# A routing count and its threshold moved half a block later in TensorE's order

## Chip, cores and metric

The kernel runs on 1 core of one Trainium2 chip. The metric is the device time in microseconds of one execution, the median over several. Engines: TensorE (PE, with PEld for its weight loads), VectorE (DVE), ScalarE (ACT), GpSimd (POOL) and SyncE (SP).

## Reference

Three stages. The first is a gated recurrence over 768 steps for 4 x 8 heads of width 40. It gives x of 3072 tokens x 320. The second routes and computes experts, the third is a two-layer network with ELU:

```python
logits = x @ w_gate                      # 3072 x 8
order = np.argsort(-logits.flatten())    # greedy, cap = 384 tokens per expert
for idx in order:
    tok, e = int(idx) // E, int(idx) % E
    if assigned[tok] >= 0 or counts[e] >= cap: continue
    assigned[tok] = e; counts[e] += 1
...
out[mask] = np.maximum(x[mask] @ w1[e], 0.0) @ w2[e]      # 320 -> 1024 -> 320
...
h = x @ w_in                                              # 320 -> 2048
g = np.where(h > 0.0, h, np.exp(np.minimum(h, 0.0)) - 1.0)
return (g @ w_out).astype(np.float32)                     # 2048 -> 320
```

## The kernel before

The recurrence (first 183 us or so of the execution) is untouched by the change. After it, the experts are filled one after another: each turn k of 0 to 7 finds the expert that is full next, computes its 384 tokens through both networks, and meanwhile does the routing for the turns behind it. "First expert" is turn 0, "steady" turns are the others. `after` is min(7 - k, 2), so that `after == 2` holds for k = 0 to 5.

A turn has two halves. In the first, TensorE does `up` and `down` for 8 blocks of 128 hidden features (W1, W2). In the second it runs over f = 0 to 18. Block f does `up2(k, f)` for f below 16 (eight products of 384 columns with the two parts of w_in, into a bank of PSUM) and, three blocks behind, `down2(k, f - 3)` (nine products of 320 columns with the two parts of w_out, from `gl_hi` and `gl_lo`). In between, `up2`'s output passes ScalarE (`elu_tanh` and `elu_exp`: relu L1681, tanh L1684, exponential L1693), VectorE (`elu`: L1503, L1506), ScalarE again (`elu_hi`: L1700, gl_hi) and GpSimd (`elu_lo`: L1243, gl_lo). `up2(k, f)` waits for `elu(k, f - 2)`, `down2(k, f - 3)` for `gl_lo` of its own block.

The routing for turn c + 1 = k + 2 is a search for a threshold, in six rounds, which runs inside these blocks:

- a comparison on VectorE (`cmp`): for the first round in six slices (`compare_first`, L849), laid behind `elu` of f = 0 to 4; for later rounds `round_compare` (L1326).
- a count on TensorE: `count_takers` (L1768), 24 products of 8 columns into bank 7.
- a test on VectorE (`round_test`: L1339, L1341), which gives `feas`.
- the spreading of the threshold on TensorE: `count_thresholds` (L1788), one product.
- the move of the threshold on VectorE (`round_move`, L1348, writes `base`), and then the next round's comparison.

Rounds 2 to 5 use `count_parts` (L1774) and `fold_parts` (L1782) instead of one count. Each engine executes its instructions in the order in which its function writes them out by hand, and waits on semaphores where data come from another engine. A wait holds everything behind it on that engine. `count_beside(k)` is the block at which the first round's count and spreading stand: 7 for the first expert, 5 for steady ones.

Of the kernel before, what the change touches and what calls it, by code (L numbers as in the profile page):

```python
# [956 lines left out]
def experts(nc, ctx, sem, bank, t, pieces, tables, E, G, CAP, DM, FF, FF2, XK):  # L957
# [155 lines left out]
    def first_expert(k):  # L1113
        return isinstance(k, int) and k == 0
# [58 lines left out]
    def count_beside(k):  # L1173
        return 7 if first_expert(k) else 5
# [97 lines left out]
    def _(dve):  # L1272
# [17 lines left out]
        def keys_at(k):  # L1290
            return (B - 1 + k) * KEY_STEPS
# [14 lines left out]
        def compare_first(k, part):  # L1306
            n = G // SLICES
            ins = tables.first_compare(dve, tables.ramp1_p, slice(part * n, part * n + n), n, keys_at(k))
            if part == SLICES - 1:
                ins.then_inc(cmp_ok, 1)  # L1310
# [24 lines left out]
        def round_test(k, q):  # L1335

            n = STEPS[q - 1][1]
            dve.wait_ge(count_pe, k * ROUNDS + q)
            nc.vector.tensor_tensor(over[0:n, :], pR[0:n, 0:E], rem[0:n, :], ALU.is_ge).then_inc(r_step, 1)  # L1339
            dve.wait_ge(r_step, did(k))  # L1340
            nc.vector.tensor_reduce(feas[0:n, :], over[0:n, :], AX.X, ALU.max).then_inc(feas_ok, 1)  # L1341
# [198 lines left out]
        def body(k, s, n, after):  # L1540

            c = k + 1
            for u in range(2, NF):
                if first_expert(k):
                    if u == 2:
                        finish_round(1, 1)
                        round_compare(1, 2)
                        round_parts(1, 2)
                        hidden(0, 2)
                        round_test(1, 2)  # L1550
                        round_move(1, 2)
                        round_compare(1, 3)
                    elif u == 3:
                        round_parts(1, 3)
                        hidden(0, 3)
                        round_test(1, 3)
                        round_move(1, 3)
                        round_compare(1, 4)
                        finish_round(1, 4)
                        round_compare(1, 5)  # L1560
                    elif u == 4:
                        round_parts(1, 5)
                        hidden(0, 4)
                        round_test(1, 5)
                        round_move(1, 5)
                        round_compare(1, 6)
                        finish_round(1, 6)
                        choose_counts(1)
                    elif u == 5:
                        choose_expert(1)  # L1570
                        hidden(0, 5)
                    elif u == 6:
                        choose_ties(1)
                        hidden(0, 6)
                    else:
                        hidden(0, 7)
                        choose_leave(1)
                        choose_close(1)
                    continue
                if after:  # L1580
                    if u == 2:
                        choose_counts(c)
                    elif u == 3:
                        choose_expert(c)
                    elif u == 4:
                        choose_ties(c)
                    elif u == 5:
                        choose_leave(c)
                        choose_close(c)
                    elif u - 6 in range(2):  # L1590
                        choose_spots(c, 2 * (u - 6))
                        choose_spots(c, 2 * (u - 6) + 1)
                hidden(k, u)
            if after == 2 and not first_expert(k):
                choose_start(c + 1)
            between_layers(k)
            for f in range(NF2):
                q, odd = (f - rounds_behind(k)) // 2 - 1, f % 2
                if after == 2:
                    if f == 0:  # L1600
                        if first_expert(k):
                            choose_start(c + 1)
                        choose_keys(c + 1)
                    if f == count_beside(k):
                        round_test(c + 1, 1)
                    elif f == count_beside(k) + 1:
                        round_move(c + 1, 1)
                        round_compare(c + 1, 2)
                    if q >= 2 and odd:
                        if q in FOLDED:  # L1610
                            round_parts(c + 1, q)
                        else:
                            round_test(c + 1, q)
                    elif q > 2:
                        round_move(c + 1, q - 1)
                        round_compare(c + 1, q)
                elu(k, f)
                if after == 2 and odd and q in FOLDED:
                    round_test(c + 1, q)
                if after and not first_expert(k) and f == list_beside(k):  # L1620
                    choose_tokens(c, 1 - s, n + s)
                if after == 2:
                    for part in (SLICES_BESIDE_SPOTS if first_expert(k) else SLICES_BESIDE).get(f, ()):
                        compare_first(c + 1, part)
                if first_expert(k) and 1 <= f <= SPOTS:
                    choose_spots(c, f - 1)
                if first_expert(k) and f == list_beside(k):
                    choose_tokens(c, 1 - s, n + s)
                if TURN <= f < TURN + NJ and after:
                    columns(c, f - TURN)  # L1630
            if first_expert(k):
                round_move(c + 1, ROUNDS - 1)
                round_compare(c + 1, ROUNDS)
                hidden(c, 0)
                round_test(c + 1, ROUNDS)
                hidden(c, 1)
            elif after:
                hidden(c, 0)
                hidden(c, 1)
            if after == 2:  # L1640
                round_move(c + 1, ROUNDS)
# [116 lines left out]
    def _(pe):  # L1758
# [197 lines left out]
        def body(k, s, n, after):  # L1956
            c = k + 1
            for u in range(2, NF):
                up(k, u)
                later = 2 if first_expert(k) else 0  # L1960
                if later and u == 2:
                    count_thresholds(1, 1)
                elif later and u < 5:
                    one_round(1, 2 * u - 3)
                if after:
                    if u == 3 + later:
                        totals(c)
                    elif u == 4 + later:
                        prefix(c, 1, eqs)
                down(k, u - 2)  # L1970
                if later and u < 5:
                    one_round(1, 2 * u - 2)
                if u == 5 + later and after:
                    prefix(c, 2, mem)
            down(k, NF - 2)
            down(k, NF - 1)
            for f in range(NF2 + LAG):
                if f == 0:
                    up2_first_two(k)
                elif 1 < f < NF2:  # L1980
                    if f == LAG and after and not first_expert(k):
                        list_tokens(c)
                    up2(k, f)
                q = (f - rounds_behind(k)) // 2 - 1
                routing = after == 2 and f < NF2 + rounds_behind(k) and q >= 2
                if after == 2 and f == count_beside(k):
                    count_takers(c + 1, 1)
                    if first_expert(k):
                        list_tokens(c)
                elif routing and f % 2:  # L1990
                    (count_parts if q in FOLDED else count_takers)(c + 1, q)
                elif routing and q - 1 in FOLDED:
                    count_thresholds(c + 1, q - 1)
                if f >= LAG:
                    down2(k, f - LAG)
                if after == 2 and f == count_beside(k):
                    count_thresholds(c + 1, 1)
                elif routing and f % 2:
                    (fold_parts if q in FOLDED else count_thresholds)(c + 1, q)
                if TURN <= f < TURN + NJ and after:  # L2000
                    columns(c, f - TURN)
                if NF2 <= f < NF2 + 2 and after:
                    up(c, f - NF2)
        experts_in_turn(pe, body)


# [22 lines left out]
```

## Time and profile before

| | |
|---|---|
| median of 3 runs | 837.94 us (837.02 to 840.19) |
| the profiled execution, its own time | 841.97 us |
| its span, first to last instruction | 840.3 us |
| mean granted TensorE clock | 0.987 |
| busy: TensorE, VectorE, ScalarE, GpSimd | 794.3, 524.4, 466.6, 392.7 us |

Busy time is the time in which an engine has an instruction in execution. Matmuls overlap each other, so the distance from the start of one to the start of the next, not its duration, is what a stream of them costs. An idle time in brackets behind a row is that of the engine just before the instruction, with what ended it.

### The profile page before, as it was taken

The page shows a single profiled execution, that of the slowest core. Times are in us where ns is not written, and L with a number is a line of the kernel's source. Part 1 is how long each engine was busy: PE and PEld are TensorE (multiplying, and loading weights), DVE is VectorE, ACT ScalarE, POOL GpSimd, SP SyncE. Part 2 cuts the span into 40 slices and gives each one's busy share as a digit, 9 for nine tenths or more (in the row PEclk, how much of TensorE's full clock was granted, in tenths as well). Part 3 has the DMA queues.
Part 4 walks back from the last instruction along what each step waited for, and adds up shares of the span by engine and source line. Part 5 has one row for each costly group of instructions (what it writes and reads, how often), then busy time and mean ns, then how long its engine had stood idle before and what let it go on. Part 6 is the DMA issues. An engine that isn't in the chain of part 4 may idle for free.

```text
span 840.3 us, 17700 instructions
## 1 busy us (share of the span) xinstructions
PE 794.3 (95%) x6029; PEld 741.3 (88%) x6029; DVE 524.4 (62%) x1438; ACT 466.6 (56%) x990; POOL 392.7 (47%) x466
## 2 busy tenths in 40 slices
PE   5999999989979999999999999999999999999994
PEld 5899999987768889899989989998999899999894
DVE  5566776766768567665866585576658656542441
ACT  5445545422417663785478276728835772893672
POOL 3535454454623652465076345516552662664133
PEclk9999999999999999999999999999999999999998
DMA  4999999413410212111122201121211212121000
GB/s 78 142 154 178 151 169 171 100 57 112 124 53 26 84 48 68 46 55 55 44 69 62 69 26 60 48 68 47 71 55 45 69 48 68 47 70 39 2 1 23
DMA packets 137987, 60.96 MB, mean 73 GB/s; under 512 B 104696, under 2 KB 136184, under 8 KB 137912
## 3 DMA queue, kind: packets, MB, share of 16 engines
q1 hardware_dynamic: 135608, 52.13, 28.7%
q0 software_dynamic: 2304, 7.87, 2.9%
q8 instruction: 42, 0.69, 0.3%
q14 instruction: 33, 0.27, 0.1%
HBM read 51.67 MB, written 8.26 MB: 71 GB/s over the span
## 4 chain that ended last, share of the span: by engine, by line
PE 63%; DVE 9%; ACT 3%; issue 1%; POOL 1%; DMA 0%; ACTq 0%; POOLq 0%
PE bank L1825 7%; PE bank L1910 7%; PE bank L1826 6%; PE bank L1828 6%; PE bank L1912 6%; PE bank L1911 6%; PE bank L1830 3%; PE bank L1829 3%; PE bank L1868 3%; PE bank L1866 3%; PE bank L1867 3%; PE bank L1762 2%; DVE cmp L849 2%; DVE unit L1506 2%; DVE unit L1503 2%
## 5 line engine op out<-in xcount | busy, mean ns | idle before, releaser
L1243 POOL TENSOR_TENSOR gl_lo<-unit,gl_hi 128x384 fp32r<-128x384 f32 x128 | 130.3, 1018 | 274.3 <-ACT gl_hi L1700 274.2
L1910 PE MATMUL bank<-Wo_hi,gl_hi 128*128 128x320 f32 x384 | 125.6, 327 | 0.5 <-POOL gl_lo L1243 0.5
L1912 PE MATMUL bank<-Wo_hi,gl_lo 128*128 128x320 f32 x384 | 119.3, 311 | 0.0
L1911 PE MATMUL bank<-Wo_lo,gl_hi 128*128 128x320 f32 x384 | 119.2, 310 | 0.0
L1503 DVE SCALAR_TENSOR_TENSOR unit<-bank,unit 128x384 f32<-128x384 f32 x104 | 57.8, 555 | 84.2 <-ACT bank L1693 79.3
L1664 ACT ACTIVATE hid_hi<-bank 128x384 fp32r<-128x384 f32 x64 | 31.4, 491 | 127.5 <-PE bank L1830 127.5
L1681 ACT ACTIVATE unit<-bank 128x384 f32<-128x384 f32 x128 | 62.2, 486 | 62.8 <-PE bank L1830 53.5
L1825 PE MATMUL bank<-x_hi,Wi_hi 128*128 128x384 f32 x224 | 81.3, 363 | 2.4 <-DVE unit L1506 1.6
L1826 PE MATMUL bank<-x_hi,Wi_lo 128*128 128x384 f32 x224 | 76.6, 342 | 0.0
L1910 PEld LDWEIGHTS bank<-Wo_hi,gl_hi 128*128 128x128 f32 x384 | 73.2, 191 | 3.1 <-POOL gl_lo L1243 3.1
L1506 DVE TENSOR_TENSOR unit<-unit,bank 128x384 f32<-128x384 f32 x128 | 70.9, 554 | 4.4
L1911 PEld LDWEIGHTS bank<-Wo_lo,gl_hi 128*128 128x128 f32 x384 | 72.9, 190 | 0.0
L1912 PEld LDWEIGHTS bank<-Wo_hi,gl_lo 128*128 128x128 f32 x384 | 72.8, 190 | 0.0
L1486 DVE SCALAR_TENSOR_TENSOR hid_lo<-bank,hid_hi 128x384 fp32r<-128x384 f32 x64 | 35.4, 554 | 55.3 <-ACT hid_hi L1664 55.1
L1684 ACT ACTIVATE unit<-unit 128x384 f32<-128x384 f32 x128 | 67.3, 525 | 4.0
L1700 ACT CAST gl_hi<-unit 128x384 fp32r<-128x384 f32 x128 | 63.9, 499 | 3.9 <-DVE unit L1506 3.5
L366 POOL TENSOR_SCALAR_AFFINE_SELECT W<-W 128x512 f32<-128x512 f32 x48 | 33.3, 716 | 66.7 <-ACT W L579 66.7
L1828 PE MATMUL bank<-x_lo,Wi_hi 128*128 128x384 f32 x224 | 58.0, 340 | 0.0
L1693 ACT ACTIVATE bank<-unit 128x384 f32<-128x384 f32 x104 | 51.5, 495 | 3.0
L501 DVE TENSOR_TENSOR PW<-bank,W 128x512 f32<-128x512 f32 x48 | 30.9, 686 | 25.8 <-PE bank L649 21.1
L695 PE MATMUL bank<-v_in,PW 128*128 128x96 f32 x384 | 46.8, 275 | 0.0
L1825 PEld LDWEIGHTS bank<-x_hi,Wi_hi 128*128 128x128 f32 x224 | 42.9, 192 | 3.6 <-DVE unit L1506 3.6
(289 smaller groups left out, 2125.6 us busy)
## 6 DMA issues: line engine op xcount, KB each, us to landing
stage<-in_moe_w_dram SPq DMA_DIRECT2D x32, 320.0 KB, 2.9
stage<-in_moe_w_dram SPq DMA_DIRECT2D x32, 256.0 KB, 2.6
stage<-in_moe_w_dram SPq DMA_DIRECT2D x96, 64.0 KB, 2.4
k_in<-in_k_dram SPq DMA_DIRECT2D x24, 160.0 KB, 3.6
q_in<-in_q_dram SPq DMA_DIRECT2D x24, 160.0 KB, 4.2
o_in<-in_o_gate_dram SPq DMA_DIRECT2D x24, 160.0 KB, 4.1
v_in<-in_v_dram SPq DMA_DIRECT2D x24, 160.0 KB, 3.6
x_rows<-xt SPq DMA_DIRECT2D x24, 160.0 KB, 3.3
```

What stands on the lines that cost most here:

```text
L1243: nc.gpsimd.tensor_tensor(gl_lo[:, b, :], ex[:, b, :], gl_hi[:, b, :].bitcast(F32), ALU.subtract).then_inc(gl_ok, 1)
L1503: nc.vector.scalar_tensor_tensor(out=ex[:, b, :], in0=exp_at(f), scalar=1.0, in1=th[:, f % 2, :], op0=ALU.add, op1=ALU.mult).then_inc(em_o ...
L1506: nc.vector.tensor_tensor(ex[:, b, :], ex[:, b, :], ring[(NF + f) % 3][:, 0:CAP], ALU.max).then_inc(g_ok, 1)
L1681: nc.scalar.activation(ex[:, b, :], ring[(NF + f) % 3][:, 0:CAP], ACT.Relu, scale=-1.0).then_inc(neg_ok, 1)
L1684: nc.scalar.activation(th[:, f % 2, :], ex[:, b, :], ACT.Tanh, scale=-0.5).then_inc(th_ok, 1)
L1700: nc.scalar.copy(gl_hi[:, b, :], ex[:, b, :]).then_inc(gl_hi_ok, 1)
L1825: nc.tensor.matmul(to, w_hi[:, c, cols], x_hi[m][:, c, :], start=(c == 0), stop=False)
L1826: nc.tensor.matmul(to, w_lo[:, c, cols], x_hi[m][:, c, :], start=False, stop=False)
L1828: nc.tensor.matmul(to, w_hi[:, c, cols], x_lo[m][:, c, :], start=False, stop=False)
L1910: nc.tensor.matmul(acc[j][:, 0:DM], gl_hi[:, f % RG, t_], Wo_hi[:, f, :], start=(f == 0), stop=False)
L1911: nc.tensor.matmul(acc[j][:, 0:DM], gl_hi[:, f % RG, t_], Wo_lo[:, f, :], start=False, stop=False)
L1912: ins = nc.tensor.matmul(acc[j][:, 0:DM], gl_lo[:, f % RG, t_], Wo_hi[:, f, :], start=False, stop=(f == NF2 - 1))
```

## The change

In steady turns with `after == 2` (k = 1 to 5), the first count stands behind `down2(k, 2)` instead of ahead of it, in block f = 5, and the spreading stands in block f = 6, behind `up2(k, 6)` and ahead of `down2(k, 3)`, instead of at the end of block 5. On VectorE the test moves from ahead of `elu(k, 5)` to behind it. The move of the threshold and the comparison of round 2 keep their place, ahead of `elu(k, 6)`. The first expert keeps its order.

```diff
@@ VectorE
                     if f == count_beside(k):
-                        round_test(c + 1, 1)
+                        if first_expert(k):
+                            round_test(c + 1, 1)
                     elif f == count_beside(k) + 1:
                         round_move(c + 1, 1)
                         round_compare(c + 1, 2)
...
                     for part in (SLICES_BESIDE_SPOTS if first_expert(k) else SLICES_BESIDE).get(f, ()):
                         compare_first(c + 1, part)
+                    if f == count_beside(k) and not first_expert(k):
+                        round_test(c + 1, 1)
@@ TensorE
-                if after == 2 and f == count_beside(k):
+                if after == 2 and first_expert(k) and f == count_beside(k):
                     count_takers(c + 1, 1)
-                    if first_expert(k):
-                        list_tokens(c)
+                    list_tokens(c)
+                elif after == 2 and not first_expert(k) and f == count_beside(k) + 1:
+                    count_thresholds(c + 1, 1)
                 elif routing and f % 2:
...
                 if f >= LAG:
                     down2(k, f - LAG)
                 if after == 2 and f == count_beside(k):
-                    count_thresholds(c + 1, 1)
+                    (count_thresholds if first_expert(k) else count_takers)(c + 1, 1)
```

## Rows read from the trace of the kernel before

**Rows 1.** The page, part 1: busy us, share of span, instructions.

```profile
PE 794.3 (95%) x6029; PEld 741.3 (88%) x6029; DVE 524.4 (62%) x1438; ACT 466.6 (56%) x990; POOL 392.7 (47%) x466
```

**Rows 2.** Waits of TensorE, 330 to 700 us: total us, times, longest.

```profile
PE bank L1768 <- DVE cmp L849: 8.0, 5, 1.6
```

**Rows 3.** Chain of waits at expert 2: start us, us, what.

```profile
425.63 0.60 DVE cmp L849
...
426.28 0.76 PE bank L1768 x24
```

**Rows 4.** Timeline of expert 2, 422 to 435 us: start us, us, engine, line.

```profile
422.41 1.02 POOL L1243 TENSOR_TENSOR gl_lo<-unit,gl_hi 128x384 fp32r<-128x384 f32 x1
...
424.37 0.34 PE L1830 MATMUL bank<-x_lo,Wi_hi 128*128 128x384 f32 x1
...
425.55 0.67 DVE L849 SCALAR_TENSOR_TENSOR cmp<-hi,bank 128x508 bf16<-128x508 f32 x1
425.86 0.49 ACT L1693 ACTIVATE bank<-unit 128x384 f32<-128x384 f32 x1
...
426.28 0.76 PE L1768 MATMUL bank<-pick,cmp 128*128 128x8 bf16 x24 [1.57 <-DVE cmp L849]
...
426.90 0.39 PE L1910 MATMUL bank<-Wo_hi,gl_hi 128*128 128x320 f32 x1
...
427.27 0.16 DVE L1341 TENSOR_REDUCE feas<-over 127x1 bf16<-127x8 f32 x1
427.35 0.55 DVE L1503 SCALAR_TENSOR_TENSOR unit<-bank,unit 128x384 f32<-128x384 f32 x1
...
428.31 0.18 PE L1788 MATMUL bank<-feas,first 128*128 128x1 bf16 x1
428.34 0.42 PE L1825 MATMUL bank<-x_hi,Wi_hi 128*128 128x384 f32 x1
428.53 0.16 DVE L1348 TENSOR_SCALAR base<-bank 128x1 f32<-128x1 f32 x1
...
428.73 0.99 DVE L1326 SCALAR_TENSOR_TENSOR cmp<-hi,base,bank 128x744 bf16<-128x744 f32 x1
...
429.66 0.34 PE L1830 MATMUL bank<-x_lo,Wi_hi 128*128 128x384 f32 x1
429.83 0.31 PE L1910 MATMUL bank<-Wo_hi,gl_hi 128*128 128x320 f32 x1
...
431.11 0.49 ACT L1693 ACTIVATE bank<-unit 128x384 f32<-128x384 f32 x1
431.16 0.34 PE L1825 MATMUL bank<-x_hi,Wi_hi 128*128 128x384 f32 x1
...
434.26 0.42 PE L1825 MATMUL bank<-x_hi,Wi_hi 128*128 128x384 f32 x1
```

**Rows 5.** Timeline of TensorE: count and later up2, experts 1 and 3.

```profile
349.53 0.78 PE L1768 MATMUL bank<-pick,cmp 128*128 128x8 bf16 x24 [1.59 <-DVE cmp L849]
...
355.88 0.34 PE L1825 MATMUL bank<-x_hi,Wi_hi 128*128 128x384 f32 x1
...
501.55 0.76 PE L1768 MATMUL bank<-pick,cmp 128*128 128x8 bf16 x24 [1.59 <-DVE cmp L849]
...
507.96 0.34 PE L1825 MATMUL bank<-x_hi,Wi_hi 128*128 128x384 f32 x1
```

**Rows 6.** Windows behind the five counts: length, busy per engine, granted clock, DMA.

```profile
350.00:353.30 3.30, 3.30 (x24) 3.10 (x21) 1.62 (x6) 0.97 (x3) 2.10 (x3) 0.50 0.22 63
...
426.90:430.20 3.30, 3.30 (x27) 3.20 (x24) 2.50 (x6) 0.99 (x3) 1.97 (x3) 1.00 0.26 81
503.60:506.90 3.30, 3.30 (x13) 3.30 (x13) 1.31 (x3) 0.31 (x1) 0.53 (x1) 0.50 0.46 134
578.90:582.20 3.30, 3.30 (x28) 3.20 (x26) 2.50 (x6) 0.98 (x3) 2.00 (x3) 1.00 0.24 81
654.20:657.50 3.30, 3.30 (x29) 3.20 (x26) 2.49 (x6) 0.98 (x3) 2.00 (x3) 1.00 0.24 77
```

## The prediction

> **What bounds the kernel now.** I read the page first: TensorE is busy for 794.3 of 840.3 us [rows 1], so it is nearly always the engine that decides, and a change can win only where TensorE stands still or runs at a lower clock. The list of waits on TensorE over experts 1 to 5 and their neighbourhood (330 to 700 us) then holds a single entry: five waits of the first count (L1768) for the comparison on VectorE (L849), 8.0 us together, 1.6 us the longest [rows 2]. These five are the count that the diff moves, one for each expert from 1 to 5. Nothing else in this half of the kernel makes TensorE wait. The chain of waits agrees: at expert 2 it runs through VectorE's last comparison slice and then into the count [rows 3].
>
> The timeline of expert 2 shows why [rows 4]. The eight products of up2 for f = 5 issue their last at 424.37 us. The count is next in TensorE's order, but it needs the last slice of the comparison, which VectorE can only start at 425.55, behind its ELU work of f = 4, and which takes 0.67 us to 426.22. So the count starts at 426.28, after 1.57 us of idle time. The next item, the nine products of down2 for f = 2, needed only gl_lo of f = 2, which GpSimd had finished at 422.41 + 1.02 = 423.43. It is ready work standing behind a wait.
>
> A second loss sits right behind the wait. At experts 1 and 3 the granted clock is 0.50 (1.2 GHz) for some 3.3 us after it, and at experts 2, 4 and 5 it stays at 1.00 (2.4 GHz) in the same place [rows 6]. From the start of the count to the start of up2 for f = 7 are 431.16 - 426.28 = 4.88 us at expert 2, but 355.88 - 349.53 = 6.35 at expert 1 and 507.96 - 501.55 = 6.41 at expert 3 [rows 4, 5]. A fall thus costs 1.5 us.
>
> **The count, moved behind down2.** No instruction is added or removed. There are 24 count products, one spreading product, the nine of down2 and eight of up2 before and after, and no DMA is issued by the moved steps. What changes is the order. down2 for f = 2 would start 0.17 us behind the last product of up2 (the distance from 429.66 to 429.83), at 424.54, and its input has been there for 1.1 us. A down2 takes 431.16 - 429.83 = 1.33 us from its first start to that of the next stage [rows 4]. So TensorE is through with it at 425.87, its last product drains to about 426.0, and the count still starts at 426.28: VectorE's slice is not touched by the move. About 0.26 us of the 1.57 us wait remain, and up2 for f = 6 follows at 426.90, where down2 started before. The move is worth 1.33 us per expert: the whole down2, since it lies inside the wait.
>
> **The spreading, moved behind up2 of f = 6.** It now waits for the test on VectorE, and the test is moved behind ELU of f = 5. Before, VectorE stood idle in front of the test, and ELU of f = 5 (whose exponential was ready at 425.86 + 0.49 = 426.35) began only at 427.35. Now ELU starts at about 426.4 and takes at most the 1.18 us between 427.35 and 428.53, to 427.6. The count is done at 427.04 and waits for no one. Test and reduction take what they take now, 427.27 + 0.16 - 427.04 = 0.39 us, so the flag is there at 427.96. up2 for f = 6 runs 429.83 - 428.34 = 1.49 us from 426.90 to 428.39. The spreading is then 0.43 us behind its flag and waits for nothing. Its own cost, 0.03 us on TensorE (428.31 to 428.34), is unchanged [rows 4].
>
> **What the moved spreading makes late.** On VectorE the move of the threshold (L1348) and the second comparison (L1326) stand ahead of ELU of f = 6, and are queued behind a result that now comes later relative to up2. Threshold: 428.39 + 0.22 (428.31 to 428.53 now) = 428.61. The comparison starts 0.20 later and takes 0.99: done at 429.80. Everything on ScalarE for f = 6 follows up2's end, now 428.34 - 426.90 = 1.44 us sooner, so its exponential ends at 431.60 - 1.44 = 430.16. The comparison is out of the way 0.36 us before ELU could begin. If it were not, ELU ending at 430.16 + 1.18 = 431.34 would still be early for its reader, up2 for f = 8, at 434.26 - 1.33 = 432.93: another 1.59 us of cover. The second count, behind up2 of f = 7 (at about 431.2), finds its comparison done for 1.4 us. So this half of the edit costs nothing, with that cover. Bounds: nothing below, and above it the 1.33 us it could at most give back per expert before it does harm [rows 4].
>
> **Sum.** 5 x 1.33 = 6.65 us. up2 for f = 7 then starts at 426.28 + 0.62 + 1.49 + 0.03 + 1.41 = 429.83 instead of 431.16 (0.62 from the count's to the next start, 1.41 for a down2 behind small products, 426.90 to 428.31): the same 1.33, by another way.
>
> **The clock.** Both falls follow the longest quiet stretch of TensorE in the block: 1.59 us idle, then 24 products of 8 columns [rows 5, 6]. Behind the change only about 0.26 us of idle time stands ahead of the count, so I expect these falls to go: 2 x 1.5 = 3.0 us in the profiled execution, 0 if they stay. For that execution, 841.97 us (its span of 840.3 and 1.67 around it), the sum is 6.65 + 3.0 = 9.65, giving 832.3. The timed median is 837.94, 4.0 lower, and its three runs spread over 3.17 us, about two falls. So a timed run has probably fewer falls than the profiled one. I take one, between the bounds of none and two: 837.94 - 6.65 - 1.5 = 829.8. With none to save it is 831.3, with two 828.3.
>
> The Trainium skill, "TensorE: Matmul & The Clock Gate", What's actually happening, calls the throttled clock the default that activity releases, and the two levels in the rows are its two. But its section "Why this matters for your kernels" warns only of idle gaps longer than any of these five. Read so, the falls were not due to these waits and would stay: 831.3, the first rival.
>
> **Rivals.** (1) The falls stay or were not in the timed runs: 837.94 - 6.65 = 831.3. For it: three of the five waits had no fall. Against: both falls came right behind this wait. (2) The saved time is given back at the next wait, because ELU and gl_lo cannot follow a TensorE that is never idle. Then the wait moves to up2 or down2 of f = 7 or 8, and the result is 837.94, or 836.4 with one fall less. For it: the exponential of f = 6 ends at 431.60 and ELU 1.18 later, 3.1 us behind the last product of its up2 (429.66), more than the 1.49 + 1.33 = 2.8 us of one block on TensorE. Against: its reader comes two blocks later, VectorE stands idle from 429.72 to 431.6, and the covers worked out above are 0.4 to 1.6 us [rows 4]. (3) Slower: VectorE, in order, stands at the threshold's move in front of ELU of f = 6, and up2 for f = 8 starves. The result would have to reach VectorE 0.36 + 1.59 + 1.33 = 3.28 us later than I reckon to eat the gain, and 0.84 us more in each of the five experts to be 0.5% slower: 842.1. It takes 0.22 us now, so little speaks for it. (4) The change does nothing, as down2 would wait for gl_lo of f = 2 as long as the count does for its comparison. It decides from 1.1 us of lateness; 837.9, and counted with (2).
>
> **How the numbers follow.** Forecast 0.72; rival 1: 0.18; rivals 2 and 4: 0.07; rival 3: 0.03. The forecast and rival 1 together span 828.3 to 831.3 by the number of falls; with the spread of a median of such runs, some 1 us below and 1.7 us above for a part given back, the range is 827.3 to 833.0. Half a per cent is 4.2 us, about what the measurement can tell from no change, so faster means below 833.7. The forecast and rival 1 are faster: 0.90; rivals 2 and 4 within: 0.07; rival 3 slower: 0.03.
>
> **What would show it.** Right: five waits of L1768 for L849 of about 0.25 us, 1.3 us in all instead of 8.0; down2 of f = 2 starting 0.17 us behind up2; no wait at L1788; no wait of up2 or down2 for f = 7 and 8; ELU of f = 5 about 0.95 us sooner after its comparison slice; the granted clock at 1.00 throughout experts 1 to 5. Wrong: down2 of f = 2 waiting for gl_lo, VectorE reaching ELU of f = 6 later than its exponential, the first count later than 0.06 us behind the comparison, or a fall of the clock still behind the count.

## The result, and the profile after

| | before | after |
|---|---|---|
| median | 837.61 us (837.02 to 840.19, 4 runs) | 830.02 us (828.95 to 830.4, 4 runs) |
| profiled execution, its own time | 841.97 us | 828.95 us |
| its span | 840.3 us | 827.2 us |
| mean granted TensorE clock in it | 0.987 | 0.996 |

The ratio after to before is 0.9901, with a 95% interval of 0.9879 to 0.9924: 7.6 us faster. The forecast started from 837.94 (three runs) and took 8.15 us off. With the fourth run the median before is 837.61, and 7.59 us came off.

The line numbers of VectorE and GpSimd named here stay, TensorE's and ScalarE's are three higher after the change: the count is L1771 (was L1768), the spreading L1791 (was L1788), up2 L1828 to L1833, down2 L1913 to L1915.

The waits of TensorE in the kernel after, 330 to 690 us (total us, times, longest), which answer to [rows 2]:

```profile
PE bank L1771 <- DVE cmp L849: 1.4, 5, 0.3
```

Still one entry, still five times, but 1.4 us in all where it was 8.0. Its first place, expert 1, in the timeline of the kernel after (start us, us, engine, line), which answers to [rows 4]:

```profile
342.10 1.02 POOL L1243 TENSOR_TENSOR gl_lo<-unit,gl_hi 128x384 fp32r<-128x384 f32 x1
...
344.04 0.34 PE L1833 MATMUL bank<-x_lo,Wi_hi 128*128 128x384 f32 x1
...
344.21 0.31 PE L1913 MATMUL bank<-Wo_hi,gl_hi 128*128 128x320 f32 x1
...
345.23 0.68 DVE L849 SCALAR_TENSOR_TENSOR cmp<-hi,bank 128x508 bf16<-128x508 f32 x1
345.38 0.31 PE L1915 MATMUL bank<-Wo_hi,gl_lo 128*128 128x320 f32 x1
...
345.97 0.76 PE L1771 MATMUL bank<-pick,cmp 128*128 128x8 bf16 x24 [0.28 <-DVE cmp L849]
...
346.08 0.56 DVE L1503 SCALAR_TENSOR_TENSOR unit<-bank,unit 128x384 f32<-128x384 f32 x1 [0.17 <-ACT bank L1696]
...
346.58 0.42 PE L1828 MATMUL bank<-x_hi,Wi_hi 128*128 128x384 f32 x1
...
347.33 0.17 DVE L1341 TENSOR_REDUCE feas<-over 127x1 bf16<-127x8 f32 x1
...
348.08 0.18 PE L1791 MATMUL bank<-feas,first 128*128 128x1 bf16 x1
348.12 0.39 PE L1913 MATMUL bank<-Wo_hi,gl_hi 128*128 128x320 f32 x1
...
348.31 0.16 DVE L1348 TENSOR_SCALAR base<-bank 128x1 f32<-128x1 f32 x1 [0.81 <-PE bank L1791]
...
348.51 0.99 DVE L1326 SCALAR_TENSOR_TENSOR cmp<-hi,base,bank 128x744 bf16<-128x744 f32 x1
...
349.52 0.34 PE L1828 MATMUL bank<-x_hi,Wi_hi 128*128 128x384 f32 x1
...
349.89 0.56 DVE L1503 SCALAR_TENSOR_TENSOR unit<-bank,unit 128x384 f32<-128x384 f32 x1 [0.39 <-ACT bank L1696]
```

down2 of f = 2 starts 0.17 us behind the last product of up2 (344.04 to 344.21) and fills the hole. Its gl_lo had been there since 342.10 + 1.02 = 343.12. The count still starts 0.06 us behind the end of the slice (345.23 + 0.68 = 345.91). The idle time ahead of it is 0.28 us. The spreading waits for nothing: its flag is there at 347.50, it starts at 348.08. From the count to up2 of f = 7 it is 349.52 - 345.97 = 3.55 us.

How much each expert gained is read best from one count to the next. Two rows of the kernel after, experts 1 and 3, on TensorE's timeline:

```profile
345.97 0.76 PE L1771 MATMUL bank<-pick,cmp 128*128 128x8 bf16 x24 [0.28 <-DVE cmp L849]
...
493.90 0.76 PE L1771 MATMUL bank<-pick,cmp 128*128 128x8 bf16 x24 [0.27 <-DVE cmp L849]
```

That is (493.90 - 345.97) / 2 = 73.97 us per expert. Before, where the clock stayed up, it is 501.55 - 426.28 = 75.27 us [rows 4, 5]. The move took 1.30 us out of each expert, 6.5 us out of five.

The two profiled spans differ by 13.1 us, much more than the medians. Most of the rest goes with the clock. Before, the fall at experts 1 and 3 cost 1.5 us each [rows 4, 5, 6], and three more falls stood in parts that the change leaves alone. Windows of the kernel before (the number behind the engines is the granted clock):

```profile
22.40:25.60 3.20, 3.20 (x16) 2.85 (x17) 0.16 (x1) 2.22 (x5) 0.69 (x2) 0.50 0.41 49
278.40:281.70 3.30, 3.30 (x12) 3.10 (x12) 2.38 (x7) 0.07 (x1) 0.04 (x1) 0.50 0.44 139
182.80:186.10 3.30, 3.30 (x12) 3.30 (x12) 2.20 (x11) 0.72 (x1) 0.52 (x2) 0.50 0.64 199
```

and the same stretches in the kernel after, with the clock up in all three:

```profile
22.40:25.60 3.20, 2.35 (x21) 2.14 (x22) 0.54 (x2) 2.42 (x5) 0.99 (x2) 1.00 0.40 44
183.00:186.30 3.30, 3.30 (x23) 3.14 (x23) 2.23 (x12) 0.47 (x1) 0.58 (x2) 1.00 0.62 197
276.00:279.30 3.30, 3.29 (x22) 3.03 (x21) 2.59 (x7) 1.19 (x3) 0.26 (x1) 1.00 0.51 139
```

The first moved count comes 349.53 - 345.97 = 3.56 us earlier than before, all of it won ahead of the first instruction that the change moves. The fall at 22.4 us has no share in it: behind the recurrence the products with `Wi_hi` (L1762, after the change L1765) start at 182.56 before and at 182.82 after. The first count behind them comes at 187.52 and 186.19, so the fall at 182.8 cost 0.26 + 1.33 = 1.6 us. By the first expert's count the lead is 276.03 - 273.81 = 2.22 us, which is 0.9 more, and whose cause was not followed. The last 1.34 us come in the stretch with the fall at 278.4. So 13.1 = 3.56 (ahead of the change) + 6.5 (the move) + 3.0 (the falls at experts 1 and 3). How much of a timed run's gain is falls is a question of its own, which the experiments take up.

### The profile page after: what moved, and what is told of

Same layout as the page of the kernel before. It is cut to its first block, busy times and chain, and to the rows that moved or that the text cites. A ratio compares the mean times of both kernels' runs of the same rounds, so it can differ in the third digit from the quotient of the medians.

```text
span 827.2 us, 17700 instructions
## 1 busy us (share of the span) xinstructions
PE 787.0 (95%) x6029; PEld 733.8 (89%) x6029; DVE 524.2 (63%) x1438; ACT 467.4 (56%) x990; POOL 393.4 (48%) x466
## 4 chain that ended last, share of the span: by engine, by line
PE 63%; DVE 6%; ACT 5%; issue 2%; POOL 1%; DMA 0%; ACTq 0%; POOLq 0%
PE bank L1828 7%; PE bank L1913 7%; PE bank L1829 6%; PE bank L1831 6%; PE bank L1915 6%; PE bank L1914 6%; PE bank L1833 3%; PE bank L1832 3%; PE bank L1869 3%; PE bank L1871 3%; PE bank L1870 3%; PE bank L1765 2%; PE bank L1857 1%; DVE unit L1506 1%; PE bank L1854 1%
## 5 line engine op out<-in xcount | busy, mean ns | idle before, releaser
L1913 PE MATMUL bank<-Wo_hi,gl_hi 128*128 128x320 f32 x384 | 124.8, 325 | 0.6 <-POOL gl_lo L1243 0.6
L1915 PE MATMUL bank<-Wo_hi,gl_lo 128*128 128x320 f32 x384 | 118.6, 309 | 0.0
L1828 PE MATMUL bank<-x_hi,Wi_hi 128*128 128x384 f32 x224 | 80.2, 358 | 2.4 <-DVE unit L1506 1.6
L1913 PEld LDWEIGHTS bank<-Wo_hi,gl_hi 128*128 128x128 f32 x384 | 72.5, 189 | 3.1 <-POOL gl_lo L1243 3.1
L1915 PEld LDWEIGHTS bank<-Wo_hi,gl_lo 128*128 128x128 f32 x384 | 72.1, 188 | 0.0
L945 POOL TENSOR_TENSOR W_lo<-stage,W_hi 128x512 fp32r<-128x512 f32 x32 | 41.4, 1293 | 9.4 <-ACT W_hi L936 9.3
```

Of the source, the lines that this page charges most:

```text
L1828: nc.tensor.matmul(to, w_hi[:, c, cols], x_hi[m][:, c, :], start=(c == 0), stop=False)
L1913: nc.tensor.matmul(acc[j][:, 0:DM], gl_hi[:, f % RG, t_], Wo_hi[:, f, :], start=(f == 0), stop=False)
L1915: ins = nc.tensor.matmul(acc[j][:, 0:DM], gl_lo[:, f % RG, t_], Wo_hi[:, f, :], start=False, stop=(f == NF2 - 1))
```

## Experiments

The kernels below ran in sets of four, each set on a chip of its own, beside the kernel before. A median alone tells little here: in the second set one unchanged kernel spread from 836.72 to 845.31 us. Most of that goes with the mean granted clock of the run. Over the 157 runs whose clock is on record (all but the four of the kernel before in the first table), a straight line with one slope and an offset for each kernel gives 6.3 us more for a mean clock lower by 0.01, and leaves 0.9 us of scatter. The table gives the median, the mean over runs of the granted clock, the time that this line gives at a mean clock of 0.990, and from the trace the distance from one expert to the next at full clock (between the moves of the first round's threshold, L1348). The 75.29 us of the kernel before are from its first trace; the values of hole_longer have falls in them.

| kernel | runs | median us | ratio to before, 95% | clock | us at 0.990 | us per expert |
|---|---|---|---|---|---|---|
| before, set 1 | 23 | 840.62 | | 0.990 | 839.8 | 75.29 |
| count_only, set 1 | 12 | 834.61 | 0.9925 (0.9896 to 0.9955) | 0.991 | 835.1 | 74.47 |
| spread_only, set 1 | 12 | 839.97 | 1.0003 (0.9974 to 1.0032) | 0.990 | 840.1 | 75.28 |
| slice_before, set 1 | 6 | 830.33 | 0.9884 (0.9845 to 0.9923) | 0.991 | 831.4 | 73.63 |
| slice_after, set 1 | 6 | 829.31 | 0.9876 (0.9833 to 0.9920) | 0.989 | 829.7 | 73.52 |
| before, set 2 | 23 | 841.07 | | 0.989 | 839.9 | |
| after_again, set 2 | 6 | 832.67 | 0.9918 (0.9890 to 0.9946) | 0.989 | 832.6 | 73.98 |
| fill_before, set 2 | 12 | 840.60 | 1.0009 (0.9986 to 1.0032) | 0.989 | 840.0 | 75.29 |
| delay1, set 2 | 6 | 829.85 | 0.9896 (0.9862 to 0.9930) | 0.992 | 832.5 | 73.98 |
| delay3, set 2 | 12 | 838.04 | 0.9976 (0.9953 to 0.9999) | 0.992 | 840.2 | 75.53 |
| before, set 3 | 11 | 837.13 | | 0.992 | 839.5 | |
| hole_longer, set 3 | 6 | 849.15 | 1.0139 (1.0108 to 1.0170) | 0.983 | 845.5 | 77.2 to 77.7 |
| hole_filled, set 3 | 6 | 844.82 | 1.0080 (1.0051 to 1.0109) | 0.991 | 845.5 | 76.44 |
| test_first, set 3 | 6 | 831.88 | 0.9926 (0.9899 to 0.9954) | 0.989 | 831.5 | 73.97 |
| slice_again, set 3 | 6 | 829.97 | 0.9907 (0.9877 to 0.9936) | 0.990 | 830.6 | 73.51 |

The changed kernel as first measured (830.02, mean clock 0.995) comes out at 833.0 by the same line, after_again at 832.6. Against before, at one clock, that is 7 us, close to the 6.5 of the traces.

**The change in two halves: count_only.**

```diff
 VectorE, against the changed kernel
-                        if first_expert(k):
-                            round_test(c + 1, 1)
+                        round_test(c + 1, 1)
...
-                    if f == count_beside(k) and not first_expert(k):
-                        round_test(c + 1, 1)
 TensorE
-                elif after == 2 and not first_expert(k) and f == count_beside(k) + 1:
-                    count_thresholds(c + 1, 1)
...
-                    (count_thresholds if first_expert(k) else count_takers)(c + 1, 1)
+                    if not first_expert(k):
+                        count_takers(c + 1, 1)
+                    count_thresholds(c + 1, 1)
```

> The count stands behind down2 of f = 2 as in the changed kernel, but the spreading follows it at once, in block 5, and VectorE's test stays ahead of ELU of f = 5. Theory (the gain is the down2 laid into the wait, and the spreading had to go half a block later to keep it): TensorE waits for the test behind the count, about 0.4 us idle and 0.6 us from start to start, so 0.7 of the 1.33 us per expert remain, 3.6 us in all: 834.0 without a change in clock falls, 833 to 834. A wait of L1788 for L1341 of about 0.4 us shows in five places. Rival (the move of the spreading is idle detail): as the changed kernel, 830.0.

Measured: 834.61 us, 74.47 us per expert, so 0.82 of the 1.31 us remain (0.7 was expected). VectorE's test has its old place here too, which test_first below shows to be without effect. TensorE's waits in this kernel, 330 to 720 us:

```profile
PE bank L1788 <- DVE feas L1341: 2.3, 5, 0.5
PE bank L1768 <- DVE cmp L849: 1.4, 5, 0.3
```

The count's wait is as short as in the changed kernel, and a new one of 0.46 us stands five times at the spreading. The second half of the edit is there to keep the first half's gain.

**spread_only.**

```diff
 TensorE, against the changed kernel
-                if after == 2 and first_expert(k) and f == count_beside(k):
+                if after == 2 and f == count_beside(k):
                     count_takers(c + 1, 1)
-                    list_tokens(c)
+                    if first_expert(k):
+                        list_tokens(c)
...
-                if after == 2 and f == count_beside(k):
-                    (count_thresholds if first_expert(k) else count_takers)(c + 1, 1)
+                if after == 2 and first_expert(k) and f == count_beside(k):
+                    count_thresholds(c + 1, 1)
```

> The count keeps its old place ahead of down2 of f = 2; only the spreading goes behind up2 of f = 6 and the test behind ELU of f = 5. Theory: nothing is gained and nothing lost, 837.6 within 1 us, five waits of 1.6 us for the comparison as before. Rival (VectorE's freed order is what pays, since ELU of f = 5 no longer stands behind the test): several us faster. Rival (the late threshold holds up ELU of f = 6): slower by some 1 us per expert.

Measured: ratio 1.0003, 75.28 us per expert where the clock stayed up, and the five waits of before (8.0 us, 5 times). The later spreading and the freed VectorE give nothing by themselves and cost nothing. (The time of 837.6 that was expected is missed by the level of this set, whose kernel before stood at 840.62.)

**test_first**, the changed kernel with VectorE's old place for the test:

```diff
 VectorE, against the changed kernel
-                        if first_expert(k):
-                            round_test(c + 1, 1)
+                        round_test(c + 1, 1)
...
-                    if f == count_beside(k) and not first_expert(k):
-                        round_test(c + 1, 1)
```

> The changed kernel with VectorE's test of the first round back ahead of ELU of f = 5. Theory (that place matters to no one, because ELU of f = 5 has its reader a block later and the flag is wanted only behind up2 of f = 6): VectorE waits for the count 0.7 us again, TensorE does not; period from expert to expert 73.98 us as in the changed kernel. Rival (VectorE's idle time is what the change removed): 1 us per expert slower.

Measured: 73.97 us per expert, as in the changed kernel, and the waits of TensorE are the same 1.4 us in five places. ELU of f = 5 had room; where the test stands on VectorE is free.

**Another cure for the same wait: slice_before and slice_after.** The same line in the kernel before and in the changed one:

```diff
-    SLICES_BESIDE = {0: (0,), 1: (1,), 2: (2,), 3: (3, 4), 4: (5,)}
+    SLICES_BESIDE = {0: (0,), 1: (1,), 2: (2,), 3: (3, 4, 5)}
```

> The order of before, but the last slice of the first comparison stands on VectorE ahead of ELU of f = 4 instead of behind it, where VectorE stood idle 0.49 us. Theory (the wait's length is set by when VectorE ends the last slice, and nothing else holds TensorE there): the slice ends at about the same time as up2 of f = 5, the wait goes down to 0.1 us or less, ELU of f = 4 is 0.2 us later, which no one waits for. Gain 1.57 to 1.7 us per expert, 8 us, and the clock falls behind the waits go: 829.6 without a share for the falls, 828.2 with one. Rival (ELU of f = 4 is itself on the path): a new wait of 0.2 us or more on up2 of f = 6 and less gained.

> The changed kernel with the same earlier slice. Theory: the 0.28 us left of each of the five waits go too, with the 0.16 us in which the last product only drains: 1.4 to 2.0 us better than 830.0, so 828.0 to 828.6, the same as the order of before with that slice, since a count that waits for nothing can stand on either side of down2. Rival (both remedies add up): 5 us or more below 830.0.

Measured: 73.63 and 73.52 us per expert, 1.66 and 1.77 less than before. In both the list of TensorE's waits between 330 and 690 us is without the count. The timeline of slice_before at expert 1:

```profile
344.19 1.86 DVE L849 SCALAR_TENSOR_TENSOR cmp<-hi,bank 128x508 bf16<-128x508 f32 x3
...
345.97 0.55 DVE L1503 SCALAR_TENSOR_TENSOR unit<-bank,unit 128x384 f32<-128x384 f32 x1
346.11 0.76 PE L1768 MATMUL bank<-pick,cmp 128*128 128x8 bf16 x24
```

The last of the three slices runs where VectorE stood idle 0.49 us, ELU of f = 4 follows it at once, and the count starts 0.06 us behind the slice with no idle time on TensorE in the view. So the wait is one of VectorE's order, and both cures reach the same loss. They do not add up: per expert it is 1.77 us against 1.31 and 1.66, and at one clock 10.1 us (8.9 in slice_again) against 7 and 8.4.

The 0.11 us per expert between the two slice kernels were expected to be nothing. Their rows show them. slice_before:

```profile
345.66 0.34 PE L1829 MATMUL bank<-x_hi,Wi_hi 128*128 128x384 f32 x1
345.84 0.34 PE L1830 MATMUL bank<-x_lo,Wi_hi 128*128 128x384 f32 x1
```

slice_after:

```profile
347.68 0.31 PE L1914 MATMUL bank<-Wo_lo,gl_hi 128*128 128x320 f32 x1
347.83 0.31 PE L1915 MATMUL bank<-Wo_hi,gl_lo 128*128 128x320 f32 x1
347.98 0.76 PE L1771 MATMUL bank<-pick,cmp 128*128 128x8 bf16 x24
```

In slice_before the count starts at 346.11, 0.27 us behind the last product of up2, where one product follows the other in 0.17 to 0.18. It still starts 0.06 us behind its slice, which ends 0.1 us too late. In the other experts the distance is 0.28 to 0.43 us. In slice_after the count starts 0.15 us behind the last product of down2, the step of that stream, in all five. A wait of 0.1 us does not show as idle time, since the product ahead of it is still in execution.

> The changed kernel with the earlier slice once more, on another set of runs. From its first profile: 73.5 us from expert to expert against 73.98 of the changed kernel, so 0.46 x 5 = 2.3 us better at the same clock; ratio to before 0.988.

Measured: 73.51 us per expert and 829.97 us. By the trace this kernel is 0.46 us per expert, 2.3 us in all, better than the changed one. The ratios to before (0.9876 and 0.9907, against 0.9901 and 0.9918) overlap, so timing does not yet separate the two. The ratio of 0.988 that was expected here came as 0.9907.

> The changed kernel again, on the same chip as the three runs below: 830.0 within 1 us.

Measured: 832.67 us, 2.6 above the first median, with a mean clock of 0.989 against 0.995, so the expectation of 830.0 within 1 us failed. The period is 73.98 both times (73.97 to 74.02).

**How much room stands behind the later threshold: delay1 and delay3.** Against the changed kernel, with 1 or 3 extra operations, whose result is not used:

```diff
                         round_compare(c + 1, 2)
+                        if not first_expert(k):
+                            for part in range(3):
+                                nc.vector.scalar_tensor_tensor(
+                                    out=spot[:, part * (G // SPOTS):(part + 1) * (G // SPOTS), :],
+                                    in0=row[:, 0:G // SPOTS]..., scalar=STEPS[0][0], in1=tables.ramp1[:, :]...,
+                                    op0=ALU.mult, op1=ALU.is_equal)
```

> The changed kernel with one more VectorE operation of 0.95 us, whose result is not used, between the second comparison and ELU of f = 6 in the five experts. Theory (0.36 us until ELU's exponential is there, and 1.59 us more until up2 of f = 8 asks for it, cover this place): ELU of f = 6 is 0.6 us later and TensorE waits for nothing, 830.0 within 1 us. Rival (the chain through ELU is already tight): up to 0.6 us per expert, 833.

Measured: 73.98 us per expert and no new wait, 829.85 us. ELU of f = 6 starts 1.77 us behind the second comparison's start (348.46 to 350.23) instead of 1.38 (348.51 to 349.89), and no one feels it.

> The same with three such operations, 2.84 us. Theory: 2.84 less the cover of 1.95 us comes through, 0.9 us per expert, 4.5 us in all: 834.5, with a wait of TensorE in block 7 or 8. Rival (the cover is much larger, since one late ELU is caught up later): 830 to 831. Rival (no cover): 844.

Measured: 75.53 us per expert, 1.55 more than the changed kernel where 0.9 were expected. The waits of TensorE, 330 to 720 us, and the rows of expert 1:

```profile
PE bank L1791 <- DVE folded_parts L1333: 7.3, 5, 1.5
PE bank L1777 <- DVE cmp L849: 1.4, 5, 0.3
```

```profile
350.24 0.99 DVE L1326 SCALAR_TENSOR_TENSOR cmp<-hi,base,bank 128x744 bf16<-128x744 f32 x1
...
351.14 3.51 DVE L1612 SCALAR_TENSOR_TENSOR spot<-row,ramp 128x768 f16<-128x768 f32 x3
...
352.09 1.74 POOL L1243 TENSOR_TENSOR gl_lo<-unit,gl_hi 128x384 fp32r<-128x384 f32 x1 [1.80 <-ACT gl_hi L1709]
...
354.57 0.54 DVE L1503 SCALAR_TENSOR_TENSOR unit<-bank,unit 128x384 f32<-128x384 f32 x1
355.15 0.55 DVE L1506 TENSOR_TENSOR unit<-unit,bank 128x384 f32<-128x384 f32 x1
...
355.62 0.18 DVE L1333 CAST folded_parts<-bank 128x32 f16<-128x32 f32 x1
...
355.87 0.26 PE L1791 MATMUL bank<-folded_parts,fold 128*128 128x8 f16 x4 [1.47 <-DVE folded_parts L1333]
```

Two things were off. The three operations took 3.51 us, not 2.84, as one of them met GpSimd's. And the first to starve is not up2 of f = 8 but the folding of the second count at the end of block 7, whose input VectorE makes only behind ELU of f = 6. ELU of f = 6 starts 354.57 - 350.24 = 4.33 us behind the comparison's start, 2.95 more than in the changed kernel, and 1.55 of it come through. So ELU had 1.40 us of room, where the prediction had 1.59 with another reader.

**The clock: fill_before, hole_longer, hole_filled.** fill_before puts products, whose results are not used, into the wait of the kernel before:

```diff
                 if after == 2 and f == count_beside(k):
+                    if not first_expert(k):
+                        pe.wait_ge(g_ok, k * NF2 + f - 1)
+                        for _ in range(8):
+                            nc.tensor.matmul(ring[(NF + f + 1) % 3][:, 0:CAP], Wi_hi[:, 0, 0:P], Wi_hi[:, 1, 0:CAP],
+                                             start=True, stop=True)
                     count_takers(c + 1, 1)
```

> The kernel of before, with 8 products of 384 columns into a free bank ahead of each of the five counts; their results are not used. They lie inside the wait (8 x 0.175 = 1.40 us of 1.57 us), so TensorE is busy where it stood idle. Theory (the two clock falls come from these idle stretches): no fall behind the five counts, the wait shrinks to 0.2 us or less without any gain of its own, and the median comes down by the falls alone, 0 to 3 us, most likely 1.5: 836.1. Rival (the falls have nothing to do with the waits): falls of 0.50 still behind some of the five counts, 837.6.

Measured: in the profiled execution the wait is 0.2 us each (1.0 in all), the period 75.29 as before, and no fall stands behind any of the five counts, while spread_only, with the waits of before, has two again (0.50 at 346.40 and at 500.00 us). But the timed runs are no faster: 840.60 against 841.07, ratio 1.0009, mean clock 0.989 in both (each within about 0.001). One fall per run fewer would have been 1.5 us, and the lower end of the interval (0.9986) leaves room for 1.2. The expectation on the median failed.

hole_longer makes the wait of before longer by one more VectorE operation ahead of the last slice, hole_filled fills it:

```diff
+                    if f == 4 and not first_expert(k):
+                        nc.vector.scalar_tensor_tensor(out=spot[:, 0:G // SPOTS, :], ...)   # as in delay1
                     for part in (SLICES_BESIDE_SPOTS if first_expert(k) else SLICES_BESIDE).get(f, ()):
                         compare_first(c + 1, part)
...
-                        for _ in range(8):     # fill_before
+                        for _ in range(13):    # hole_filled
```

> The kernel of before with one more VectorE operation of about 0.95 us, whose result is not used, ahead of the last slice of the first comparison in the five experts: each of the five waits becomes 2.5 us instead of 1.57. Theory (a quiet stretch of TensorE brings the clock down, and it is a matter of its length): nearly all five are followed by a granted clock of 0.50, against two of five before; from 836 at a steady clock it is 836 + 5 x 0.95 + 5 x 1.5 = 848, and with the falls that a timed run has elsewhere about 851, the mean clock some 0.006 below that of before. Rival (the falls come on their own, wherever TensorE stands): 845.5 and the mean clock of before.

> The same with 13 products of 384 columns into a free bank ahead of each of the five counts, results not used, 2.3 of the 2.5 us. Theory (quiet stretches make the falls): the same length of wait, but no fall behind it: 844 to 845.5, mean clock as before or above, 6 us faster than its twin without the filling. Rival (the falls come on their own): the same time as its twin.

Measured: 849.15 and 844.82 us, mean clocks 0.983 and 0.991. At one clock they are equal (845.5), so the whole difference is clock. It is 4.3 us where 6 were expected. The waits of hole_longer, its count at expert 1, and its windows around the five counts:

```profile
PE bank L1773 <- DVE cmp L849: 13.6, 5, 2.7
...
347.18 0.34 PE L1835 MATMUL bank<-x_lo,Wi_hi 128*128 128x384 f32 x1
350.24 0.81 PE L1773 MATMUL bank<-pick,cmp 128*128 128x8 bf16 x24 [2.72 <-DVE cmp L849]
...
349.60:352.90 3.30, 2.66 (x31) 2.67 (x32) 1.93 (x5) 0.93 (x2) 2.77 (x3) 0.50 0.02 6
353.00:356.20 3.20, 3.20 (x12) 3.00 (x11) 1.15 (x2) 0.00 (x0) 0.00 (x0) 0.50 0.46 132
427.00:430.30 3.30, 1.16 (x28) 1.17 (x29) 2.42 (x6) 2.38 (x5) 3.30 (x4) 1.00 0.16 45
506.60:509.80 3.20, 3.20 (x13) 3.00 (x12) 2.25 (x5) 0.00 (x0) 1.06 (x2) 0.50 0.42 118
585.10:588.30 3.20, 3.20 (x13) 3.00 (x12) 1.70 (x3) 0.00 (x0) 0.48 (x1) 0.50 0.42 126
659.00:662.00 3.00, 0.66 (x25) 0.67 (x25) 2.28 (x3) 2.56 (x6) 3.00 (x3) 1.00 0.21 57
```

Three of the five waits of 2.7 us have a fall. At experts 3 and 4 it comes 1.0 and 1.6 us behind the start of the count. At expert 1 the clock is down from 349.6 us on, 0.6 us before the count starts, so there the idle time alone stood right ahead of the fall. In hole_filled none of the five has one:

```profile
350.00:353.00 3.00, 3.00 (x21) 2.90 (x20) 2.13 (x4) 0.45 (x1) 0.96 (x1) 1.00 0.39 123
...
500.00:503.00 3.00, 2.53 (x36) 2.21 (x36) 2.12 (x5) 1.91 (x5) 3.00 (x4) 1.00 0.04 15
577.00:580.00 3.00, 2.51 (x37) 2.19 (x35) 2.08 (x6) 1.38 (x4) 3.00 (x3) 1.00 0.00 0
```

So an idle stretch of TensorE can bring the clock down, and keeping it busy there prevents it: at 2.7 us this is shown, in trace and in time. Nearly all five were expected, three came.

The other traces say something on the shorter waits. Between 330 and 700 us the granted clock is 0.99 in the kernel before and in spread_only, with two falls in each, at four of their ten waits of 1.6 us. In all nine traces of kernels in which the wait is 0.3 us or gone, in fill_before and in hole_filled it is 1.00: no fall at any of 55 counts. So in the traces the falls of this part go with TensorE's idle time at 1.6 us too. Ahead of 330 us, where no kernel here differs, a trace has between none and three falls.

## Why the prediction held

The time, 830.02 us, is 0.2 from the 829.8 forecast. That it is so close is luck: the fall counted for a timed run has no support, the median before came 0.33 us lower with its fourth run, and the same kernel gave 832.67 us on another chip. The mechanism, a down2 laid into the wait five times, is what was forecast. For the profiled execution 832.3 was forecast and 828.95 measured; the 3.56 us won ahead of the change are more than the difference.

**The count behind down2.** Right. 1.33 us per expert were forecast, 1.30 measured; 0.26 us of wait were to remain, 0.28 did; down2 starts 0.17 us behind up2, the count 0.06 behind the slice. spread_only shows that without this half nothing is won, and slice_before that the wait hung on VectorE's last slice alone.

**The spreading behind up2 of f = 6.** Right. It was to be 0.43 us behind its flag (0.58 in the trace) and to wait for nothing. count_only shows the price of leaving it: 0.49 us per expert.

**VectorE's order.** That ELU of f = 5 would start some 0.95 us sooner was right, and test_first shows that it is worth nothing.

**What the later threshold makes late.** The conclusion was right, the second term not. The 0.36 us ahead of ELU are 0.39 in the trace. The 1.59 us behind them, counted to up2 of f = 8, are 1.40, to the folding of the second count (delay3). I had followed the operation's own reader and passed over what stands next on VectorE, the cast for TensorE's fold.

**The clock.** The profiled execution lost its falls at experts 1 and 3, as forecast: 3.0 us, and 6.5 + 3.0 = 9.5 us for the changed part against 9.65 reckoned. The one fall (1.5 us) that I took for a timed run has no such support. The median came down by 7.59 us, of which 6.5 are the move, so 1.1 are left, within what the interval of the ratio (about 1.9 us either way) leaves open. fill_before says that removing the quiet stretch of 1.57 us alone moves neither the median nor the mean clock by as much as one fall, and after_again has the mean clock of the kernel before beside it, 0.989. The chain "idle, then a fall" is shown for waits of 2.7 us, in trace and time. For the 1.57 us of this kernel it is shown in the traces alone: four of ten waits had a fall (before, spread_only), none of 55 counts with a short or filled wait. The timed runs do not show it. How often these waits have a fall there stays open, and so does the split of the last 1.1 us. The Trainium skill, "TensorE: Matmul & The Clock Gate", What's actually happening, calls the throttled clock the default that activity releases: hole_longer and hole_filled agree, 0.50 at three of five quiet stretches and 1.00 at all filled ones. The Trainium skill, same page, "Why this matters for your kernels", warns of idle gaps longer than these. Here falls came with waits of 1.59 and 2.7 us, so the first rival, that the falls at these waits would stay, did not hold in the trace.

**The rivals.** That the saved time would be given back at the next wait has nothing for it: no other wait of TensorE appeared in five experts. The slower case needed a result 3.28 us later than reckoned. delay3 made ELU of f = 6 2.95 us later and gave back 1.55 of it, which took away more than the whole gain per expert: 75.53 against 75.29 us. The 3.28 us are 0.39 + 1.40 + 1.31 = 3.10 by the runs.

## What to carry to other kernels

Where the engine that bounds a kernel waits for a small result, look at what stands next in its order: work whose inputs have long been there is worth its full length if laid into the wait, up to the length of the wait (here 1.3 of 1.57 us). Then move the consumer of the small result by the same half block, or a new wait appears behind it (0.46 us in count_only). Read the other side of the wait too: here moving one slice on VectorE ahead of an operation that was not ready yet removes all of it with one line. And for the room behind a moved result, count every instruction behind it on the engine that waits, not only the reader you had in mind.

## What the runs showed of the hardware

- The granted clock sets the spread of this kernel: over 157 runs, 6.3 us for 0.01 of the mean clock. A kernel measured at 830.02 us with a mean clock of 0.995 gave 832.67 at 0.989, with the same 73.98 us per expert. The period in the trace is the steadier measure for changes of some us.
- Between 330 and 700 us of the 14 traces, every fall of the granted clock to 0.50 stands at a TensorE wait of 1.6 us (four of ten) or 2.7 us (three of five). None stands at the 55 counts whose wait was 0.5 us or less, with or without filling.
- A VectorE operation of 768 elements with both inputs in SBUF took 0.95 us alone in delay1. In delay3, where it met GpSimd's operations, three of them took 3.51 us, the last 1.77, and GpSimd's gl_lo took 1.74 instead of 1.02 us. The ELU and comparison operations, of which one input lies in PSUM, overlap the same GpSimd operations at their usual 0.55 and 0.67 us (in the changed kernel the comparison at 345.23 took 0.68 us beside gl_lo at 344.65, which took 1.02). The Trainium skill, "SBUF — State Buffer", SBUF: two separate sides, tells of a port pair that VectorE and GpSimd share and that an operation with two SBUF inputs takes; the rows fit.
